# Windowed attention in groups of four blocks instead of three, ahead of two fused feed-forward layers

## The reference, cut to what matters

```python
# q, k, v: (4, 8, 576, 64)
rel = pos[:, None] - pos[None, :]
mask = (rel >= 0) & (rel < 64)                      # causal, window of 64
attn = softmax(where(mask, q @ k.T / 8, -1e9)); a = attn @ v
x = a.transpose(0, 2, 1, 3).reshape(2304, 512)
xn = x / sqrt(mean(x * x) + 1e-6) * rms_g           # per token
x = (silu(xn @ w_gate) * (xn @ w_val)) @ w_out      # 512 -> 1536 -> 512
h = relu(x @ w_in); out = (h * h) @ w_down          # 512 -> 2048 -> 512
```

## Time and profile before

| | us |
|---|---|
| median of 3 runs (lowest, highest) | 904.03 (903.77, 904.55) |
| the profiled execution, its span | 904.36, 902.6 |
| TensorE busy in the span | 887.2 |
| VectorE, ScalarE, GpSimd busy | 565.5, 484.7, 580.0 |
| granted TensorE clock, mean | 1.000 |

### The profile page before, as it was taken

How to read it: one execution, slowest core, us unless ns; L and a number is a source line. 1 busy time by engine, 2 the same in 40 slices (tenths; PEclk the granted TensorE clock), 3 DMA queues, 4 the chain that set the end, 5 groups by cost and what they waited for, 6 DMA issues and landing times.

```text
span 902.6 us, 14709 instructions
## 1 busy us (share of the span) xinstructions
PE 887.2 (98%) x5356; PEld 880.6 (98%) x5356; DVE 565.5 (63%) x795; ACT 484.7 (54%) x872; POOL 580.0 (64%) x562
## 2 busy tenths in 40 slices
PE   7999899999999999999999999999999999999998
PEld 6989799999999999999999999999999999999998
DVE  6776667647856655855556867767377675577222
ACT  3887766654566554455554445454355453455332
POOL 7897749757378858358868458573377553485332
PEclk9999999999999999999999999999999999999999
DMA  9985222212222222222222122211422222420122
GB/s 233 247 219 156 59 65 71 71 53 59 82 69 73 70 59 59 60 82 72 77 63 68 61 77 71 76 59 59 140 75 81 56 59 68 149 70 20 57 70 94
DMA packets 105943, 76.98 MB, mean 85 GB/s; under 512 B 24464, under 2 KB 88976, under 8 KB 105872
## 3 DMA queue, kind: packets, MB, share of 16 engines
q1 hardware_dynamic: 105872, 76.05, 29.6%
HBM read 71.31 MB, written 4.72 MB: 84 GB/s over the span
## 4 chain that ended last, share of the span: by engine, by line
PE 93%; POOL 2%; DVE 2%; ACT 1%; issue 1%; DMA 0%; SPq 0%; POOLq 0%
PE bank L610 29%; PE bank L612 29%; PE bank L611 29%; PE bank L562 2%; PE bank L585 2%; POOL wide L459 1%; POOL probs L465 1%; PE bank L571 1%; ACT acts L802 0%; DVE acts L1070 0%; DMA q_diag<-in_qT 0%; PE bank L604 0%; PE bank L595 0%; POOL sq L474 0%; DVE bank L1111 0%
## 5 line engine op out<-in xcount | busy, mean ns | idle before, releaser
L610 PE MATMUL bank<-xc_hi,w_hi 128*128 128x384 f32 x844 | 282.7, 335 | 1.2 <-ACT acts L802 1.0
L612 PE MATMUL bank<-xc_hi,w_lo 128*128 128x384 f32 x844 | 282.0, 334 | 0.0
L611 PE MATMUL bank<-xc_lo,w_hi 128*128 128x384 f32 x844 | 282.0, 334 | 0.0
L610 PE MATMUL bank<-hs_hi,d_hi 128*128 128x384 f32 x672 | 225.3, 335 | 0.1
L612 PE MATMUL bank<-hs_hi,d_lo 128*128 128x384 f32 x672 | 224.6, 334 | 0.0
L611 PE MATMUL bank<-hs_lo,d_hi 128*128 128x384 f32 x672 | 224.5, 334 | 0.0
L507 POOL TENSOR_TENSOR d_lo<-d_raw,d_hi 128x512 fp32r<-128x512 f32 x84 | 127.4, 1517 | 149.7 <-ACT d_hi L802 149.7
L1198 DVE TENSOR_TENSOR hs_lo<-h,hs_hi 128x768 fp32r<-128x768 f32 x84 | 83.7, 997 | 137.4 <-ACT hs_hi L802 137.2
L610 PEld LDWEIGHTS bank<-xc_hi,w_hi 128*128 128x128 f32 x844 | 158.5, 188 | 1.5 <-issue 1.5
L611 PEld LDWEIGHTS bank<-xc_lo,w_hi 128*128 128x128 f32 x844 | 158.5, 188 | 0.0
L612 PEld LDWEIGHTS bank<-xc_hi,w_lo 128*128 128x128 f32 x844 | 158.4, 188 | 0.0
(11 more groups left out here) (88 smaller groups left out, 1225.1 us busy)
## 6 DMA issues: line engine op xcount, KB each, us to landing
d_raw<-in_w_down SPq DMA_DIRECT2D x48, 256.0 KB, 2.6
w_raw<-in_w_gate SPq DMA_DIRECT2D x36, 256.0 KB, 2.9
w_raw<-in_w_val SPq DMA_DIRECT2D x72, 128.0 KB, 2.8
d_raw<-in_w_out SPq DMA_DIRECT2D x36, 256.0 KB, 2.6
w_raw<-in_w_in SPq DMA_DIRECT2D x24, 256.0 KB, 2.7
w_raw<-in_w_in SPq DMA_DIRECT2D x48, 128.0 KB, 2.6
k_sb<-in_kT SPq DMA_DIRECT2D x16, 288.0 KB, 4.3
q_diag<-in_qT SPq DMA_DIRECT2D x32, 144.0 KB, 4.7
```

The source lines that it names most:

```text
L610: pe.matmul(ps, w_h, v_h, start=first, stop=False, skip_group_check=joined)
L611: pe.matmul(ps, w_h, v_l, start=False, stop=False, skip_group_check=joined)
L612: return pe.matmul(ps, w_l, v_h, start=False, stop=last, skip_group_check=joined)
```

## The change

- `GU` = 4: 36 groups of four blocks over the running number of the block, so a group can hold blocks of two sequences (9 is no multiple of 4). `runs_of(g)` gives the stretches of one sequence within a group; an output copy is issued per stretch and head, so 12 groups have four copies instead of two. Waits for loads and the first-block mask move into the loop over blocks.
- `valid` is BF16 (was float32) and holds nine patterns in place of four; GpSimd copies patterns 4 to 8 from the first ones. VectorE waits for the first `VALID` constants before slot 0 and for all before slot 1.
- `wide` lies where `d_hi` and `d_lo` are; 5 `probs` buffers instead of 6.
- GpSimd widens a group in the slot in which it scales it (its stream has the same order; an addition of squares now follows the widening).
- The side jobs have other slot numbers (`diagonals` 29; the others stand in the diff), and the products of the first feature step lie in slots 35 to 40.
- Loads of sequence 0: keys and the second query half go from ScalarE's queue, the first half from SP's; each half is cut behind the fourth block. SP issues sequence 1 only when keys and the first four blocks of both halves have landed (`first_in`).
- `down_low` of a layer's first chunk goes ahead of `h_b` in GpSimd's stream.

```diff
-CONSTS = 20
+VALID, CONSTS = 14, 22
 
 
 SEQS = KT * BATCH
-GU = 3
-GPS = NBLK // GU
+BLOCKS = SEQS * NBLK
+GU = 4
 GW = GU * P
-BODY = KT * GPS
-GROUPS = SEQS * GPS
-S_LAG, N_LAG, E_LAG, T_LAG, PV_LAG, O_LAG = 1, 2, 3, 4, 5, 6
+GROUPS = BLOCKS // GU
+S_LAG, N_LAG, T_LAG, PV_LAG, O_LAG = 1, 2, 4, 5, 6
 TAIL = GROUPS + O_LAG
-PR = 6
+PR = 5
 ER = 3
 QR = 3
 VR = 3
+PATTERNS = "EOEOEEOEO"
...
+def last_group(seq):
+
+    return (seq * NBLK + NBLK - 1) // GU
+
+
+def blocks(g):
+
+    return [divmod(n, NBLK) for n in range(g * GU, (g + 1) * GU)]
+
+
+def pattern(g):
+
+    return PATTERNS.index("".join("EO"[b % 2] for _, b in blocks(g)))
+
+
+def runs_of(g):
+
+    runs = []
+    for u, (seq, b) in enumerate(blocks(g)):
+        if runs and runs[-1][2] == seq:
+            runs[-1][1] += 1
+        else:
+            runs.append([u, 1, seq, b])
+    return runs
+
+
+O_DONE = [2 * sum(len(runs_of(n)) for n in range(g)) for g in range(GROUPS + 1)]
+A_GROUP = ((KT - 1) * NBLK + NT // WIN - 1) // GU
+B_GROUP = ((2 * KT - 1) * NBLK + (PW - SEQ) // WIN - 1) // GU
...
-        valid, at = place("valid", [P, 4, 2, WIN], F32, at)
+            wide.append(sb(f"wide{n}", [P, GU, 2, WIN], F32, d_at + n * GW * 4))
+        valid, at = place("valid", [P, len(PATTERNS), 2, WIN], BF16, at)
...
-                    sp.wait_ge(qk_done, GPS * (i - QR + 1))
+                    sp.wait_ge(qk_done, last_group(i - QR) + 1)
...
-                    sp.wait_ge(pv_done, GPS * (i - VR + 1))
+                    sp.wait_ge(pv_done, last_group(i - VR) + 1)
...
-            load_qk(0)
+            sp.dma_start(q_diag[0][0:WIN, 0:GU, 0:WIN], first_rows(0, slice(0, GU))).then_inc(first_in, 16)
+            sp.dma_start(q_diag[0][0:WIN, GU:NBLK, 0:WIN], first_rows(0, slice(GU, NBLK))).then_inc(qk_in[0], 16)
+            sp.wait_ge(first_in, 48)
...
-                if 0 <= g - E_LAG < GROUPS:
-                    n = g - E_LAG
-                    pool.wait_ge(scaled, n + 1)
-                    if n >= ER:
-                        pool.wait_ge(tr_done, n - ER + 1)
-                    nc.gpsimd.tensor_tensor(wide[n % ER][:], probs[n % PR][:, :, 0:WIN].unsqueeze(2).broadcast_to(
-                        [P, GU, 2, WIN]), valid[:, n % GPS % 2:n % GPS % 2 + GU, :, :], ALU.mult).then_inc(widened, 1)
                 if 0 <= g - N_LAG < GROUPS:
                     n = g - N_LAG
                     v = probs[n % PR][:, :, 0:WIN]
                     pool.wait_ge(inverted, n + 1)
                     nc.gpsimd.tensor_tensor(v, v, sums[:, n % PR, :].unsqueeze(2).broadcast_to([P, GU, WIN]),
                                             ALU.mult).then_inc(scaled, 1)
-                for c, adds in ((0, (20, 22, 24)), (1, (30, 31, 32))):
+                    if n >= ER:
+                        pool.wait_ge(tr_done, n - ER + 1)
+                    pool.wait_ge(scaled, n + 1)
+                    k = pattern(n)
+                    nc.gpsimd.tensor_tensor(wide[n % ER][:], v.unsqueeze(2).broadcast_to([P, GU, 2, WIN]),
+                                            valid[:, k:k + GU, :, :], ALU.mult).then_inc(widened, 1)
+                for c, adds in ((0, (16, 18, 20)), (1, (24, 25, 26))):
...
+                    if u == U0[q] - 1:
+                        down_low(M0[r])
...
+                    for u, (seq, b) in enumerate(blocks(g)):
+                        par = seq % QR
+                        ps = s_ps[g % 2][:, u * P:(u + 1) * P]
+                        if b == 0:
+                            if seq > 0:
+                                pe.wait_ge(qk_in[par], 48 * (seq // QR + 1) - (16 if par == 0 else 0))
+                            if seq < QR:
+                                pe.wait_ge(q_zero, 2 * par + 2)
+                            pe.matmul(ps, ident_bf[:], first_mask[:], start=True, stop=False)
                         m = b // 2
 
                         step = EVEN if b % 2 or b == 0 else EVEN - 1
                         keys = k_sb[par][:].rearrange("p (n c) -> p n c", c=WIN)[:, m:m + step + 1:step, :]
-                        mm = pe.matmul(s_ps[g % 2][:, u * P:(u + 1) * P], q_diag[par][:, b, :],
-                                       keys, start=b > 0, stop=True)
+                        mm = pe.matmul(ps, q_diag[par][:, b, :], keys, start=b > 0, stop=True)
...
-                if g == 33:
+                if g == 27:
                     token_sums(0, bank[0])
-                if g == 40:
+                if g == 30:
                     spread(0, bank[0:2])
-                if g == 46:
+                if g == 35:
                     pe.wait_ge(lo1_done, 1)
-                    pe.wait_ge(norm_done, 2 * KT)
+                    pe.wait_ge(norm_done, KT)
                     plain(0, "ga", P_A11, "B11")
-                    plain(0, "va", P_A21, "B11")
-                if g == 47:
-                    pe.wait_ge(lo2_done, 1)
+                if g == 36:
                     pe.wait_ge(x_split, split_count(0, "B21"))
                     plain(0, "ga", P_A12, "B21", ga_mm)
+                if g == 37:
+                    pe.wait_ge(lo2_done, 1)
+                    pe.wait_ge(norm_done, 2 * KT)
+                    plain(0, "va", P_A21, "B11")
                     plain(0, "va", P_A22, "B21", va_mm)
-                if g == 48:
+                if g == 38:
                     pe.wait_ge(shifted, GROUPS)
                     plain(0, "gb", P_A11, "B12")
                     plain(0, "vb", P_A21, "B12")
-                if g == 50:
+                if g == 40:
...
+            act.dma_start(k_sb[0][:], kT[0:P, :]).then_inc(first_in, 16)
+            act.dma_start(q_diag[0][WIN:P, 0:GU, WIN:P], first_rows(HD, slice(0, GU))).then_inc(first_in, 16)
+            act.dma_start(q_diag[0][WIN:P, GU:NBLK, WIN:P], first_rows(HD, slice(GU, NBLK))).then_inc(qk_in[0], 16)
...
-                    for half in range(2):
-                        to, of = output(n, half)
-                        copy(to, of, o_out)
+                    for run in runs_of(n):
+                        for half in range(2):
+                            to, of = output(n, run, half)
+                            copy(to, of, o_out)
...
-                if g in (22, 24):
-                    high1((g - 22) // 2)
-                if g in (23, 25):
-                    high2((g - 23) // 2)
-                if g == 35:
+                if g in (18, 20):
+                    high1((g - 18) // 2)
+                if g in (19, 21):
+                    high2((g - 19) // 2)
+                if g == 28:
                     root(0)
-                if g in (44, 45):
-                    x_high(0, ("B11", "B21")[g - 44], KT)
-                if g in (46, 47):
-                    x_high(0, ("B12", "B22")[g - 46], 2 * KT)
-                if g == 49:
+                if g in (33, 34):
+                    x_high(0, ("B11", "B21")[g - 33], KT)
+                if g in (36, 37):
+                    x_high(0, ("B12", "B22")[g - 36], 2 * KT)
+                if g == 38:
                     gate_plain(0, 0)
-                if g == 50:
+                if g == 40:
                     x_high(0, "T3")
-                if g == 52:
+                if g == 41:
...
-                if g == 34:
+                if g in (19, 21):
+                    low1((g - 19) // 2)
+                if g in (20, 22):
+                    low2((g - 20) // 2)
+                if g == 28:
                     mean_square(0, bank[0])
-                if g == 37:
+                if g == 29:
                     inverse(0)
-                if 41 <= g < 45:
-                    if g == 41:
+                if g in (31, 32):
+                    if g == 31:
                         dve.wait_ge(rb_mm, 1)
                         dve.wait_ge(gain_in, 16)
-                    c = (g - 41) // 2
-                    for k in range(2 * ((g - 41) % 2), 2 * ((g - 41) % 2) + 2):
-                        normalise(half_cols(0, k, c), k, bank[c][:, 0:NT])
-                if 45 <= g < 49:
-                    x_low(0, ("B11", "B21", "B12", "B22")[g - 45])
-                if g == 49:
+                    for k in (2 * (g - 31), 2 * (g - 31) + 1):
+                        normalise(half_cols(0, k, 0), k, bank[0][:, 0:NT])
+                if 33 <= g < 37:
+                    normalise(half_cols(0, g - 33, 1), g - 33, bank[1][:, 0:NT])
+                if g in (34, 35):
+                    x_low(0, ("B11", "B21")[g - 34])
+                if g in (37, 38):
+                    x_low(0, ("B12", "B22")[g - 37])
+                if g == 39:
```

More of the change, by code:

```diff
@@ L122, in build @@
         w_raw = [sb(f"w_raw{n}", [P, 8 * HALF_K], F32) for n in range(2)]
+        d_at = top[0]
         d_hi = [sb(f"d_hi{n}", [P, D], F32R) for n in range(2)]
@@ L286, in raw_part, with output @@
             return w_raw[u % 2][:, n * HALF_K:(n + count) * HALF_K]
-        def output(g, half):
-            seq, n = g // GPS, g % GPS
```

(38 more changed lines are left out.)

28 lines of the change are left out of this document (10 added, 18 removed).

## The result

The changed kernel takes 906.4 us (median of 20 runs), the one before 904.13: the ratio is 1.003, 95% interval 1.0018 to 1.0041. I had forecast 901.4 with a range of 895.8 to 906.4, and more than half the chance on faster. Its runs also spread more, from 904.6 to 911.9, where those of before lie between 903.7 and 905.9 but for one execution of 1792. The profiled execution took 906.16, with a span of 904.4.

A forecast was written before the change was run, and what follows sets the result against it. TensorE, busy 98% of the span, was taken as the bound, with gains only in attention. Its lost time, 11.0 + 3.2 + 0.2 + 0.3 + 2.4 = 17.1 against 19.75 us, gave 2.65 less: 901.4 us, range 895.8 to 906.4.

The forecast's parts named there:

- R: The point, 112.51 us in the kernel before, after which 790.1 us stay constant; forecast to come near 109.9.
- (a): Stretch from the start to slot 5: TensorE loses 11.0 us instead of 10.0, bounds 8.6 to 13.
- later loads: Queries queued behind V and 512 KB weight loads come late for the scores: 1.5 + 1.7 = 3.2 us, bounds 0 and 6.
- (b): Stretch after slot 5, to 67.44 us before: loss from late GpSimd falls from 2.9 to 0.2 us, bounds 0 to 2.9.
- (c): Stretch around the root, 67.44 to 84.56 us before: loss falls from 2.1 to 0.3 us, bounds 0 to 2.1.
- (d): Last stretch of attention, from 84.56 us before to R: loss falls from 4.8 to 2.4 us, bounds 1.0 to 4.8.
- The first loads: At the start: first matmul at 4.4 us instead of 6.23, then waits of 1.6 and 2.4 for sequences 1 and 2.
- Only issue time is saved: Rival on the second queue at the start: first matmul at 5.5, all behind it 1.1 later, 902.5 us; chance 0.12.
- the rival on it: GpSimd is slower on the BF16 mask and becomes the bound once widening passes 1.55 us: 906.4 us, chance 0.08.
- d_lo: `down_low` ahead of `h_b`: gain 0, since TensorE has no wait behind 112.5 us; bounds below 0.3.
- After R: First-layer side jobs come some 2 us later against TensorE, with 5 us of margin: cost 0, at worst 1.
- the load stream sets the pace: Rival: ordinary sequences' queries land later than 7.0 us after the V product's end and hold the scores; 907.4 us, chance 0.12.

The follow-up runs named there:

- a1: The changed kernel with V of sequence j+1, instead of j+2, loaded behind queries and keys of j+3: 900.55 us, ratio 0.9959.
- a5: The changed kernel with 48 spare, unused matmuls right before the waits for sequences 7 and 9: 905.4 us, ratio 1.0015.
- a2: The changed kernel with the two 512 KB weight loads moved behind queries and keys, V order unchanged: 902.97 us, ratio 0.9983.
- a8: a1 with `down_low` put back behind `h_b` and the weight sums, as before the change: 900.93 us, ratio 0.9967.
- a4: a1 without SP's wait for `first_in` ahead of sequence 1: 897.95 us, ratio 0.9934.
- c2: a4 with 32 spare matmuls before the first wait, and queries and keys of sequence 2 loaded ahead of V of 0 and 1: 897.18 us, ratio 0.9922.
- a6: a1 with sequence 0 loaded as before the change (uncut, all from SP, nothing held): 897.59 us, ratio 0.9936.
- a7: The changed kernel with only the old start put back (sequence 0 uncut, all from SP, nothing held): 903.15 us, ratio 0.9994.
- c1: a6 with 32 spare matmuls before the first wait: 898.22 us, ratio 0.9938.

## Why the prediction was wrong, step by step

The work ahead of R is the 92.9 us of the prediction. Lost time up to R, from the starts in the rows above and the same sums as there:

| stretch | before | predicted | measured |
|---|---|---|---|
| (a) up to slot 5 (16.83) | 10.0 | 11.0 | 11.8 |
| later loads, slots 5 to 27 | 0 | 3.2 | 7.8 |
| (b) GpSimd | 2.9 | 0.2 | 0 |
| (c) root | 2.1 | 0.3 | 0.8 |
| (d) the end | 4.8 | 2.4 | 1.0 |
| sum | 19.75 | 17.1 | 21.4 |

- **The failed step is "Later loads": "Against 7.5 and 7.0 I take 1.5 + 1.7 ... bounds 0 and 6".** The place and the sequences (7 and 9) were right. The size was not, twice. First, the waits. They are 2.93 and 2.79 us (6.2 with what restarting adds and a short one at sequence 5), where the term had 3.2. I had taken the landing times of before, 9.2 and 9.7 behind the issue of V, and then some off for less backlog. Measured were 10.3 at sequence 7 and 9.7 at sequence 9, so nothing was to come off; and the scores asked 7.3 and 6.8 us behind the V product's end, not 7.5 and 7.0. Second, the pause has a price of its own, which the term put at nothing: the 1.6 us of matmuls at the lower clock behind it (I wrote 2.2 in the expectations, with the 0.5 of the restarts and the short wait in it). Together that is the 7.8. a1 takes both away and gains 5.9; that the second is the pause's doing is supported by a5, and not settled. I had named the fall-back as a bound at the start and as 1 us in a rival, but not where the longest pauses stood. (The 5.5 us to spare that I wrote for the kernel before are 5.0: landed at 25.8, asked for at 30.8. The sum does not use it.)
- **The first loads** went as worked out: first matmul 4.54 (4.4), sequence 1 at 9.87 (9.8), sequence 2 at 15.83 (15.1). That last landing is most of the 0.8 us that (a) was short. What a single profile doesn't show is the clock behind that second pause: whole in the changed kernel's profiled execution, 0.57 to 0.61 in those of a1, a2, a5 and a8, which have the same start; each such stretch costs 1.6 us. (Ahead of it go by the spacing: in the changed kernel the 18 scores from 9.95 on take 4.13 us, a spacing of 0.22, though the granted clock is given as 1.00 there.) Such stretches are a good part of the spread of 904.6 to 911.9: the eight executions with a mean granted clock of 0.998 took 904.6 to 906.3 us, the five with 0.992 or less 906.9 to 911.9. They are not all of it, since a5 at 0.996 to 1.000 still spread from 903.0 to 910.1; a4 and c2, without these pauses, spread by 1.2 and 0.6 us.
- **The second queue.** The rival "Only issue time is saved", to which I gave 0.12, had the first matmul at 5.5. With the hold it came at 4.54, and without it at 4.90 and 5.73, near the rival. A good part of what I took for the second queue's gain was that of the hold, and the hold cost more than it gave.
- **GpSimd, the root and the end** came out as worked out or better: no wait for GpSimd, one of 0.52 us at the root, ScalarE's last copies still 0.93. These parts of the change give some 8 us against before, and a4 and a6, in which they stand without the two faults, are 6 us faster than the kernel before.
- **BF16 mask:** 1.12 us for 512 elements, 2.2 ns for one, against 2.5 in float32 at 384; the rival on it is out. **d_lo:** nothing, as said. **After R:** 790.1 again.
- Of the rivals, "the load stream sets the pace" came nearest: 907.4, of which the measured 906.4 is 1.0 short. Its point of decision, an ordinary sequence later than 7.0 us, was just not passed in the profile (sequence 5: 23.80 to 30.8, 7.0, and TensorE lost 0.2 us on it); sequences behind weights, and the slow matmuls, were enough. That its time came so near is therefore luck. I gave it 0.12 and should still have given it more, since I had written down that the ordinary ones fit by 0 to 0.5 us only.

What stays open: why the clock fell behind the pause of 2.93 us at 40 and not behind that of 2.79 us at 56, nor behind one of 3.11 us in a7; why it falls at 16 in some executions only; and why the last queries of sequence 7 took 6.8 us to land, where the same load took 5.7 before.

## What to carry to other kernels

When a pipeline's group grows, a lag of so many slots grows in work too, and each load that waits for the far end of the pipeline comes that much later against its near end. For every transfer, write down what releases it, what stands behind it in its queue, and how long before use that leaves; a load should never stand behind one whose release comes later. And price a pause of TensorE at more than its length, since it may be followed by matmuls at half speed, as seven of 13 were here. A first operation that started 1.7 us sooner was worth less than nothing here, since the next loads were held back for it.

## What the runs showed of the hardware

- Behind waits of TensorE of 1.73 to 2.93 us the granted clock was 0.57 to 0.61 over the next 4 us in seven cases, and behind waits of 1.54 to 3.11 us it was 1.00 in six: the length alone did not decide it. Behind the two waits into which 48 small matmuls were put (2.7 us of them) it was 1.00.
- With 32 of them ahead of the first scores, the first 16 score matmuls took 2.48 us (c1) where they took 3.31 without (a6); there was no gain in time, as the wait for sequence 2 came next.
- In the changed kernel, from V's issue to the landing of the last query behind it took 7.0 us for sequence 5 (23.80 to 30.8), 5.8 for 6 (28.36 to 34.2), and with 512 KB of weights between, 10.3 for 7 (33.10 to 43.4) and 9.7 for 9 (49.17 to 58.9): by the difference of the means about 3.6 us for 512 KB. In each of these cases the next V load went out before the queries had landed; what part that has is not shown.
